# Attention scores from two halves of TensorE's rows: first keys on the upper 64, last keys on the lower, three products in place of two full ones

## What is computed

```python
# attention, top_k = 32
scores = scale * np.matmul(q, k.transpose(0, 1, 3, 2))
kth = np.partition(scores, -top_k, axis=-1)[..., -top_k:-top_k + 1]
scores = np.where(scores >= kth, scores, -1000000000.0)
attn = np.exp(scores - np.max(scores, axis=-1, keepdims=True))
attn = attn / (np.sum(attn, axis=-1, keepdims=True) + 1e-09)
x = np.matmul(attn, v)            # then heads side by side: (2304, 512)
# first block: 512 -> 2048 -> 512
h = x @ w_in
x = (h * (1.0 / (1.0 + np.exp(-h)))) @ w_out
# second block: 512 -> 1024, 1024 -> 1024, 1024 -> 512
a = x @ w1
b = x @ w2
out = (a * b @ w3) @ moe2_w_out
```

## Time and profile before

| What | Value |
|---|---|
| median of 3 timed runs | 1142.83 us (1137.77 to 1145.79) |
| profiled execution, its own time | 1139.89 us |
| span in the profile | 1138.0 us |
| instructions in the span | 24334 |
| mean granted TensorE clock | 0.984 of full |
| DMA, mean | 273 GB/s |

### The profile page before, as it was taken

One profiled execution on the slowest core, in us unless ns is written; L12 is line 12 of the kernel. 1 busy time (PEld: TensorE's weight loads), 2 busy tenths in 40 slices (PEclk: granted clock), 3 DMA queues, 4 the chain that ended last, 5 costly groups with the idle time before them and its releaser, 6 DMA issues.

```text
span 1138.0 us, 24334 instructions
## 1 busy us (share of the span) xinstructions
PE 1056.2 (93%) x7872; PEld 986.5 (87%) x7872; DVE 930.9 (82%) x2066; ACT 773.0 (68%) x1921; POOL 621.1 (55%) x803
## 2 busy tenths in 40 slices
PE   1998577899999999999999999999999999999898
PEld 1554477799999999999999999999999999999897
DVE  5698886798889999999999998989999999991110
ACT  4577767677777787777767777877677767764221
POOL 3566767766665455566645555666545545543211
PEclk9999679999999999999999999999999999999999
DMA  8987769986998599779966996899579847963972
GB/s 270 316 281 250 260 221 311 310 275 200 330 374 288 163 342 346 260 233 359 359 236 212 335 345 212 265 365 362 193 249 335 297 154 279 331 216 128 312 244 93
DMA packets 129053, 310.42 MB, mean 273 GB/s; under 512 B 14240, under 2 KB 43936, under 8 KB 128928
## 3 DMA queue, kind: packets, MB, share of 16 engines
q1 hardware_dynamic: 110112, 275.30, 71.8%
q10 hardware_dynamic: 18816, 33.56, 8.4%
HBM read 263.19 MB, written 45.61 MB: 271 GB/s over the span
## 4 chain that ended last, share of the span: by engine, by line
PE 72%; DMA 9%; POOL 4%; DVE 4%; issue 4%; ACT 4%; ACTq 2%; SPq 1%; POOLq 0%; DVEq 0%
PE ps_h L1033 6%; PE ps_h L1035 6%; PE ps_h L1034 6%; DMA win<-win_split 6%; PE ps_s L929 5%; PE ps_x L965 5%; PE ps_h L995 5%; PE ps_h L996 5%; PE ps_h L997 5%; PE ps_y L1017 4%; PE ps_y L1019 4%; PE ps_y L1018 4%; PE ps_t L944 4%; PE ps_y L1046 3%; PE ps_y L1047 3%
## 5 line engine op out<-in xcount | busy, mean ns | idle before, releaser
L828 DVE MAX8 top<-rest 128x8 f32<-128x576 f32 x432 | 309.9, 747 | 0.0
L639 POOL TENSOR_TENSOR g_lo<-gate,g_hi 128x256 fp32r<-128x256 f32 x216 | 160.0, 741 | 240.7 <-ACT g_hi L796 240.2
L830 DVE MATCH_REPLACE8 rest<-top,rest 128x576 f32<-128x576 f32 x288 | 212.9, 743 | 0.5
L995 PE MATMUL ps_h<-x_hi,win 128*128 128x256 f32 x576 | 167.9, 291 | 9.1 <-DMA win<-win_split 8.9
L1033 PE MATMUL ps_h<-x_hi,w_hi 128*128 128x256 f32 x576 | 166.1, 288 | 5.1 <-DVE x_lo L884 4.4
L627 POOL TENSOR_TENSOR pT<-p_raw,pT 128x640 fp32r<-128x640 f32 x72 | 113.4, 1575 | 103.1 <-ACT pT L756 103.1
L1017 PE MATMUL ps_y<-g_hi,wout 128*128 128x256 f32 x576 | 165.7, 288 | 1.1 <-POOL g_lo L639 1.0
L996 PE MATMUL ps_h<-x_lo,win 128*128 128x256 f32 x576 | 163.0, 283 | 0.0
L997 PE MATMUL ps_h<-x_hi,win 128*128 128x256 f32 x576 | 162.9, 283 | 0.0
L1035 PE MATMUL ps_h<-x_hi,w_lo 128*128 128x256 f32 x576 | 162.7, 282 | 0.0
L1034 PE MATMUL ps_h<-x_lo,w_hi 128*128 128x256 f32 x576 | 162.7, 282 | 0.0
(11 more groups left out here) (78 smaller groups left out, 2840.2 us busy)
## 6 DMA issues: line engine op xcount, KB each, us to landing
win<-win_split SPq DMA_DIRECT2D x135, 512.0 KB, 6.4
wout<-wout_split SPq DMA_DIRECT2D x135, 512.0 KB, 4.9
wout<-w_dram SPq DMA_DIRECT2D x72, 512.0 KB, 3.9
v_split<-v_dram SPq DMA_DIRECT2D x64, 320.0 KB, 5.2
k_split<-k_dram SPq DMA_DIRECT2D x64, 288.0 KB, 5.8
v_dram<-v_split SPq DMA_DIRECT2D x32, 320.0 KB, 6.1
k_raw<-kT SPq DMA_DIRECT2D x64, 144.0 KB, 5.4
k_dram<-k_split SPq DMA_DIRECT2D x32, 288.0 KB, 6.9
```

The lines of the kernel that those rows point to most:

```text
L639: nc.gpsimd.tensor_tensor(g_lo[:, n % NR, :], gate[:, n % NG, :], g_hi[:, n % NR, :].bitcast(F32), ALU.subtract).then_inc(g_split, 1)
L828: nc.vector.max(best[:, 8 * n:8 * n + 8], sc if step == 0 else left).then_inc(topk_step, 1)
L830: nc.vector.match_replace(left, best[:, 8 * n:8 * n + 8], sc if step == 1 else left, BELOW_ALL).then_inc(topk_step, 1)
L995: nc.tensor.matmul(ps_h[:, f % 2, 0:UN], hi, xh, start=(c == 0), stop=False)
```

## The change

The keys are laid out anew. Rows 0 to 63 now belong to the first 288 keys and rows 64 to 127 to the last 288; in each of them the first 288 columns of `k_split` are `hi` and the last 288 `lo`. A score matmul uses 64 rows of the array: the upper rows with the first keys into one PSUM bank, the lower rows with the last keys into the other. A group now has three products (hi by hi, hi by lo, lo by hi) times two halves, six matmuls of form 64*128 with 288 columns, in the place of four of form 128*128; the product lo by lo is gone. In all there are 960 score matmuls where there were 640. `k_raw` needs half the columns, SP loads half the bytes, ACT casts 128x288, GpSimd subtracts 128x288, and GpSimd's waits on its own last instruction go, around the key subtraction.

```diff
-        k_raw, k_split = sb("k_raw", [P, 2, S]), sb("k_split", [P, NK, S], F32R)
+        k_raw, k_split = sb("k_raw", [P, 2, HS]), sb("k_split", [P, NK, S], F32R)
...
-                    sp.dma_start(k_raw[0:D, n % 2, :], kT[b, h]).then_inc(k_loaded[n % 2], 16)
-                    sp.dma_start(k_raw[D:P, n % 2, :], kT[b, h]).then_inc(k_loaded[n % 2], 16)
+                    for half in range(2):
+                        sp.dma_start(k_raw[D * half:D * half + D, n % 2, :],
+                                     kT[b, h][:, HS * half:HS * half + HS]).then_inc(k_loaded[n % 2], 16)
...
-            before, half_before = (p_zeroed, 1), False
             for _, op in pool_order():
                 kind = op[0]
-                if kind == "KR" or half_before:
-
-                    pool.wait_ge(*before)
-                half_before = kind == "KR"
...
                     pool.wait_ge(k_rounded, n + 1)
-                    ks = k_split[D:P, e % NK, :]
-                    nc.gpsimd.tensor_tensor(ks, k_raw[D:P, n % 2, :], ks.bitcast(F32), ALU.subtract).then_inc(k_ready, 1)
-                    before = (k_ready, n + 1)
+                    nc.gpsimd.tensor_tensor(k_split[:, e % NK, HS:S], k_raw[:, n % 2, :],
+                                            k_split[:, e % NK, 0:HS].bitcast(F32), ALU.subtract).then_inc(k_ready, 1)
...
-                    nc.scalar.copy(k_split[:, e % NK, :], k_raw[:, n % 2, :]).then_inc(k_rounded, 1)
+                    nc.scalar.copy(k_split[:, e % NK, 0:HS], k_raw[:, n % 2, :]).then_inc(k_rounded, 1)
...
-                        parts += [(q_hi[:, s % 2, at:at + P], e), (q_lo[:, s % 2, at:at + P], e)]
-                    for n, (q, e) in enumerate(parts):
+                        parts += [(q_hi, 0, at, e), (q_hi, 1, at, e), (q_lo, 0, at, e)]
+
+                    for n, (q, rest_, at, e) in enumerate(parts):
                         for half in range(2):
-                            m = nc.tensor.matmul(ps_s[:, half, 0:HS], q, k_split[:, e % NK, HS * half:HS * half + HS],
+                            rows = slice(D * half, D * half + D)
+                            m = nc.tensor.matmul(ps_s[:, half, 0:HS], q[rows, s % 2, at:at + P],
+                                                 k_split[rows, e % NK, HS * rest_:HS * rest_ + HS],
                                                  start=(n == 0), stop=(n == len(parts) - 1))
```

More of the change, by code:

```diff
@@ L572, in _ @@
                                             ALU.subtract).then_inc(q_ready, 1)
-                    before = (q_ready, s + 1)
                 elif kind == "KR":
@@ L586, in _ @@
                                             v_split[:, e % NV, :, hi_cols(h)].bitcast(F32), ALU.subtract).then_inc(v_ready, 1)
-                    before = (v_ready, n + 1)
                 elif kind == "WS":
@@ L594, in _ @@
                                             ring[:, place, 0, :].bitcast(F32), ALU.subtract).then_inc(w_ready[part], 1)
-                    before = (w_ready[part], i + 1)
                 elif kind == "W12":
@@ L601, in _ @@
                                             ALU.subtract).then_inc(w12_ready, 1)
-                    before = (w12_ready, c + 1)
                 elif kind == "BOUNDS":
@@ L614, in _ @@
                                             ALU.subtract).then_inc(bias_ready, 1)
-                    before = (bias_ready, s + 1)
                 elif kind == "NORM":
@@ L621, in _ @@
                                             ALU.mult, ALU.mult).then_inc(normed, 1)
-                    before = (normed, t + 1)
                 elif kind == "LO" and not on_vector(op[1]):
@@ L628, in _ @@
                                             pT[:, 0:KCH, cols].bitcast(F32), ALU.subtract).then_inc(p_split[t % 2], 1)
-                    before = (p_split[t % 2], t // 2 + 1)
                 elif kind == "XL":
@@ L634, in _ @@
                                             ALU.subtract).then_inc(x_split, 1)
-                    before = (x_split, q + 1)
                 elif kind == "GL":
@@ L640, in _ @@
                                             ALU.subtract).then_inc(g_split, 1)
-                    before = (g_split, n + 1)
         @block.scalar
```

## The result

The changed kernel takes 1148.6 us (median of 20 runs) where the kernel before takes 1141.6 (20 runs): a ratio of 1.0062, 95% interval 1.0047 to 1.0078. In a second set it was 1.0056 (1.0034 to 1.0078). It is slower by 0.6%, some 7 us, where 1129 was forecast. That is less than the 1% that the prediction took for the least that can be told from no change, but both intervals lie above 1.

A forecast was written before the change was run, and what follows sets the result against it. TensorE was taken to bound 240 to 1010 us one for one. From the profiled 1139.9 us, -14.1 (scores) -2 (early) +2 (VectorE) gave 1126, as a median 1129; range 1120 to 1168, the likeliest case's own 1121 to 1140.

The forecast's parts named there:

- Switching the array's form: Before and after each lane's scores, between 128*128 and 64*128: taken as costing nothing; upper bound 0.70 us a lane.
- the third rival: Drain at each form switch around scores, 0.35 us a lane, or halves not overlapping; 1168 us for the drain; chance 0.14.
- A pair costs 0.132 us: Score matmuls on TensorE: two row halves run side by side, 0.42 us a group, saving 14.1 us.
- Given back by VectorE, 2 us: VectorE, next bound with a fixed order, takes back 2 us (0 to 6) of the saving.
- Key splitting: ACT's cast 0.24 us and GpSimd's key subtraction 0.61 us shorter; 2 us (0 to 5) won in the first 240 us.
- Key loads: SP's key DMAs carry half the bytes, same count and queue places: taken as worth nothing.

The follow-up runs named there:

- extra_cols: Kernel before plus one small matmul of form 128*64 (half the columns) ahead of each lane's scores; 1148.6 us, ratio 1.0043.
- extra_rows: Kernel before plus one small matmul of form 64*128 ahead of each lane's scores; 1172.3 us; its control, the same matmul at 128*128, 1149.5 us.
- one_less: Kernel before with one of a group's four score matmuls left out, no change of form; 1126.8 us, ratio 0.9857.
- one_load: Kernel before, full-height scores, each fresh head's keys loaded once in place of twice; 1130.6 us, ratio 0.9905; second run 1135.5 us, 0.9943.
- after_full_bytes: Changed kernel with all 576 key columns loaded each time, same number of DMAs; 1152.5 us, ratio 1.0093.
- after_turns: Changed kernel with each group's three upper-row matmuls issued first, then the three lower; 1156.2 us, ratio 1.0123.

## Why the prediction was wrong

It was wrong in sign: 1129 was forecast and 1148.6 came, slower than before. One step did that.

- **Switching the array's form** ("I take nothing, the value nearest the rows"). This step failed. The nearest rows were of the tail transpose, form 128*64, and they were read rightly: extra_cols confirms that this form is free. What failed is to carry them to the form 64*128. Measured in the changed kernel are 0.38 us for the two changes of a lane, 0.30 over its control in extra_rows, where 0 was taken, 0.06 was the end of the forecast's own range and 0.70 the upper bound. The rows of before could not tell the two kinds of switch apart; the range should have been built on that, and the third rival not been put among the least likely.
- **A pair costs 0.132 us**: right. Two of a pair have one start, the second group of a lane costs 0.39, and the lower half's products are free. The weight loads of the two halves overlap as well, which the earlier trace rows could not show. With the forms free the forecast might have held: one_less saves 15.6 us where 14.1 was the term. No run has pairs and free forms together.
- **Given back by VectorE, 2 us**: the wait for VectorE grew by 1 to 1.5 us in one_less. What the term leaves out is the wait for the weights of `win`: it is 4 to 8 us longer there, and in the changed kernel 3 to 7 us shorter.
- **Key splitting**: durations right. The 2 us early are not seen by themselves: TensorE's wait for q_lo in the first 240 us is 25.7 and 25.6 us in the kernel before and 25.0 and 24.7 in the changed one.
- **Key loads, "Nothing"**: wrong in its reason. SP issues the first load of w3 behind the first keys: at 14.4 to 15.3 us in the six profiles with two full loads, at 12.4 to 13.6 in the four with halves, at 12.9 and 13.0 with one load. TensorE waits for w3 at the start. One load in place of two is worth 6 to 11 us on the whole (one_load, twice); half of the bytes perhaps 4, within the noise (after_full_bytes). All early gains together are 4 to 7 us in the changed kernel's profiles, where 2 was taken; how they part into bytes, DMA issues and GpSimd was not tried one by one.
- **The third rival** named the mechanism and the place, and its 0.35 us a lane was near the 0.38 measured. Its time, 1168, was 19 too high, because idle time took up a part of what TensorE added and because of the early gain. The gaps that it foretold at both ends of the scores (0.2) are there, 0.21 and 0.21.

The measured time lies inside the wide range (1120 to 1168), which ends at the mild end of the third rival. That is no merit of the forecast: the mechanism that came had a chance of 0.14.

The Trainium skill's rule that a change of tiling mode drains TensorE ("TensorEngine Tiling (Array Packing)", Key Properties) agrees here with half the rows (some 0.20 us a change in the changed kernel) and not with half the columns (0.01 for two); that the pause is a drain no row shows. The Trainium skill's rule on order ("TensorE: Matmul & The Clock Gate", Part 3, The mechanism), by which matmuls run strictly first in, first out, does not hold in after_turns, where lower matmuls started ahead of upper ones that stand before them in the program.

What stays open: why half the columns cost nothing, why the two changes add only 0.30 us in extra_rows, and what part of the early gain each cause has.

## What to carry to other kernels

Matmuls that use half the rows ran two at a time at the price of one, but each change between them and full-height ones cost about 0.2 us on TensorE; a visit of three pairs saved 0.13 us and paid 0.38 for its two changes. Count the visits before the products: by an estimate from these prices, a visit needs three groups of this size to break even (0.39 saved). No run had such a visit; with two groups a lane still lost some 0.12. And when a change makes a transfer smaller, look at what queues behind it at the start: loading the keys once, without the new form, was the better kernel. A time saved on the busiest engine can come back as a longer wait for the next resource, so read its own time and its idle time apart.

## What the runs showed of the hardware that was not expected

- A change between 128*128 and 64*128 costs 0.19 to 0.20 us in the changed kernel: 0.09 more until the next weight load starts, 0.11 for the load. Around one small matmul (extra_rows) two of them add 0.30. A change to 128*64 and back costs 0.01 at most.
- The two row halves take their matmuls independently over a few instructions: three upper ones followed by three lower ones ran as pairs (0.59 us), six and six did so only from the fourth on (1.37 in place of 0.99).
- One kernel's first w3 product started 5.6 us apart in two profiles (29.15 and 23.56) while the whole runs agreed within 0.2%.
